# Expert 0 with two tiles at least: tiles 0 and 1 written out ahead of the expert loop

## The reference

```python
# 1. clustered attention: q, k, v are (2, 8, 768, 64); 16 cluster centroids per head
q_assign = argmax(normalised(q) . normalised(centroids));  k_assign likewise
mask = q_assign[:, :, :, None] == k_assign[:, :, None, :]
attn = softmax(where(mask, q @ k.T / 8, -1e9));  x = (attn @ v)   # -> (1536 tokens, 512)

# 2. mixture of experts: 8 experts, w1 (8, 512, 1024), w2 (8, 1024, 512)
logits = x @ w_gate;  e_idx = argmax(logits, axis=1)
gate_w = softmax(logits)[token, e_idx];  eom = sigmoid(x @ w_output_gate)
for e in range(8):
    mask = e_idx == e
    out[mask] = gate_w * eom[mask, e] * (relu(x[mask] @ w1[e]) @ w2[e])

# 3. dense part: w_in (512, 2048), w_out (2048, 512)
h = out @ w_in;  return (h * sigmoid(1.702 * h)) @ w_out
```

## Time and profile before

| | us |
|---|---|
| time, median of 3 runs (lowest to highest) | 813.9 (813.64 to 814.22) |
| time of the profiled execution | 814.3 |
| its span | 812.8 |
| TensorE matmuls busy | 748.0 (92%) |
| TensorE weight loads busy | 639.9 (79%) |
| VectorE busy | 425.5 (52%) |
| ScalarE busy | 371.4 (46%) |
| GpSimd busy | 164.8 (20%) |

### The profile page before, as it was taken

How to read it: one execution, slowest core, us unless ns; L and a number is a source line. 1 busy time by engine, 2 the same in 40 slices (tenths; PEclk the granted TensorE clock), 3 DMA queues, 4 the chain that set the end, 5 groups by cost and what they waited for, 6 DMA issues and landing times.

```text
span 812.8 us, 12003 instructions
## 1 busy us (share of the span) xinstructions
PE 748.0 (92%) x4099; PEld 639.9 (79%) x4099; DVE 425.5 (52%) x791; ACT 371.4 (46%) x707; POOL 164.8 (20%) x254
## 2 busy tenths in 40 slices
PE   4799999999999992879999999999999999999994
PEld 3699899988988871768777878888888888888883
DVE  3587888889878763455555546453322212222221
ACT  2577777777776840456565646463111101110110
POOL 5232242222635874101010101010000100020001
PEclk9999999999999996989999999999999999999997
DMA  7672552835526535773645364250000100010001
GB/s 173 153 167 69 135 123 65 184 71 129 150 55 136 212 130 129 235 261 117 234 141 205 124 234 181 67 191 18 1 0 1 53 0 1 1 52 0 1 1 52
DMA packets 61330, 86.36 MB, mean 106 GB/s; under 512 B 32576, under 2 KB 34768, under 8 KB 60752
## 3 DMA queue, kind: packets, MB, share of 16 engines
q1 hardware_dynamic: 55728, 75.23, 32.7%
q0 software_dynamic: 3376, 6.35, 2.2%
q10 hardware_dynamic: 2160, 3.93, 1.4%
HBM read 56.01 MB, written 9.05 MB: 80 GB/s over the span
## 4 chain that ended last, share of the span: by engine, by line
PE 71%; DVE 5%; ACT 5%; issue 5%; SPq 4%; DMA 3%; POOL 3%; ACTq 2%; another core or an unknown queue 0%; POOLq 0%; DVEq 0%
PE ps L958 16%; PE ps L686 9%; PE ps L973 5%; PE ps L975 5%; PE ps L974 5%; PE ps L759 5%; PE ps L901 4%; PE ps L903 3%; PE ps L902 3%; PE ps L888 3%; SPq L394 3%; PE ps L890 3%; PE ps L889 3%; PE ps L736 2%; PE ps L732 2%
## 5 line engine op out<-in xcount | busy, mean ns | idle before, releaser
L1341 DVE TENSOR_TENSOR pt_l<-ps,pt_h 128x384 fp32r<-128x384 f32 x192 | 105.9, 552 | 41.6 <-ACT pt_h L1062 40.1
L1210 ACT ACTIVATE g<-ps 128x512 f32<-128x512 f32 x48 | 28.7, 598 | 205.4 <-PE ps L958 205.4
L1571 DVE CAST gt_h<-g 128x512 fp32r<-128x512 f32 x48 | 20.5, 427 | 179.9 <-ACT g L1210 179.9
L1062 ACT CAST pt_h<-ps 128x384 fp32r<-128x384 f32 x192 | 92.6, 483 | 43.5 <-PE ps L686 43.5
L686 PE MATMUL ps<-ident,probs 128*128 128x128 f32 x576 | 97.3, 278 | 3.9 <-DVE pt_l L1341 2.2
L1300 DVE TENSOR_REDUCE nmax<-ps 128x1 f32<-128x768 f32 x96 | 91.0, 948 | 7.2 <-PE ps L736 7.2
L1033 ACT ACTIVATE probs<-ps,nmax 128x768 f32<-128x768 f32 x96 | 87.7, 913 | 4.8 <-DVE nmax L1300 4.8
L686 PEld LDWEIGHTS ps<-ident,probs 128*128 128x128 f32 x576 | 70.8, 144 | 17.7 <-ACT probs L1033 4.2
L958 PE MATMUL ps<-x2t_h,wl 128*128 128x512 f32 x192 | 74.9, 390 | 0.1
L973 PE MATMUL ps<-wh,gt_l 128*128 128x512 f32 x192 | 74.8, 389 | 0.0
L958 PE MATMUL ps<-x2t_h,wh 128*128 128x512 f32 x192 | 74.7, 389 | 0.0
(11 more groups left out here) (197 smaller groups left out, 1451.7 us busy)
## 6 DMA issues: line engine op xcount, KB each, us to landing
raw<-in_moe_w SPq DMA_DIRECT2D x32, 1024.0 KB, 7.7
ka<-hi_t SPq DMA_DIRECT2D x32, 192.0 KB
raw<-in_moe_w_in SPq DMA_DIRECT2D x4, 1024.0 KB, 5.9
raw<-in_moe_w_out SPq DMA_DIRECT2D x4, 1024.0 KB, 6.8
xg<-xs ACTq DMA_DIRECT2D x15, 256.0 KB, 3.9
qn<-in_q SPq DMA_DIRECT2D x16, 192.0 KB, 3.8
kn<-in_k SPq DMA_DIRECT2D x16, 192.0 KB, 3.9
vn<-in_v SPq DMA_DIRECT2D x8, 384.0 KB, 5.2
```

What stands on the lines that cost most here:

```text
L1062: nc.scalar.copy(pt_h[g % 2][:, half * GT:(half + 1) * GT, t3 * P:(t3 + 1) * P], ps[:, 4 + half, 0:GQ].rearrange("p (c n) -> p c n", c=GT) ...
L1341: nc.vector.tensor_tensor(pt_l[g % 2][at_p], ps[:, 4 + half, 0:GQ].rearrange("p (c n) -> p c n", c=GT), pt_h[g % 2][at_p].bitcast(F32), AL ...
```

## The change

Expert 0's minimum for the tiles after its first becomes one, so that it has two tiles always. With that, tile 0 and the first layer of tile 1 need no counts: they are written out straight on TensorE, ScalarE and VectorE with constant rows, and the loop starts at expert 1 (or at expert 0's third tile). The counts' chain is cut in parts (`count_tiles`, `region_rows`, `dense_rows`) that are put between VectorE's other work, each with a semaphore (`g_tiles`, `g_region`, `g_rows`). The pads have a semaphore for each expert; SP writes pad 0, fetches tile 1 by a constant row, writes pads 1 and 2, and the others one by one in the loop. POOL fetches tile 0's gate weights during attention (`first_info`). The second set of rank matmuls stands inside tile 0's first layer, and its totals have a bank column and a semaphore of their own (`g_total`).

```diff
@@ -340,16 +345,16 @@
         def expert_loop(eng, counter, tile, only=None):
 
             for e in range(E):
-                n = eng.value_load(ntiles[0:1, e:e + 1], min_val=1, max_val=MAXT)
-                tile(eng.snap(counter) if e else None, e, 0)
+                n = eng.value_load(ntiles[0:1, e:e + 1], min_val=1 if e else 2, max_val=MAXT)
                 if e:
+                    tile(eng.snap(counter), e, 0)
                     eng.reg_add(counter, counter, 1)
-                if only is not None:
-                    with eng.If(n < 2):
-                        only(e)
-                with eng.If(n > 1):
-                    tile(eng.snap(counter), e, 1)
-                    eng.reg_add(counter, counter, 1)
+                    if only is not None:
+                        with eng.If(n < 2):
+                            only(e)
+                    with eng.If(n > 1):
+                        tile(eng.snap(counter), e, 1)
+                        eng.reg_add(counter, counter, 1)
                 with eng.If(n > 2):
                     with eng.Fori(2, n):
                         tile(eng.snap(counter), e, 2)
...
             def fill(e):
 
                 n = sp.value_load(filled[0:1, e:e + 1], min_val=0, max_val=N)
-                return sp.dma_start(xs[bass.ds(n + e * REGION, TILE), :], zeros[:, :])
-
+                sp.dma_start(xs[bass.ds(n + e * REGION, TILE), :], zeros[:, :]).then_inc(s_pad[e], 16)
+
+            sp.wait_ge(g_filled, 1)
+            fill(0)
+            sp.wait_ge(s_pad[0], 16)
+            sp.wait_ge(s_disp, 16 * NT)
+            sp.dma_start(xg[:, :], xs[TILE:2 * TILE, :]).then_inc(xg_in, 16)
+            fill(1)
+            sp.wait_ge(pv_done, PAIRS * NG)
+            sp.wait_ge(g_rows, 1)
+            fetch_second(1)
+            fill(2)
             sp.wait_ge(g_tiles, 1)
-            row = sp.value_load(region_row[0:1, 2:3], min_val=0, max_val=E * REGION)
-            sp.wait_ge(s_disp, 16 * NT)
-            for e in range(2):
-                fill(e).then_inc(s_first, 16)
-            sp.wait_ge(s_first, 48)
-            fetch(row)
-            for e in range(2, E):
-                fill(e).then_inc(s_fill, 16)
-            sp.wait_ge(pv_done, PAIRS * NG)
-            fetch_second(1)
             tiles = sp.alloc_register("sp_tiles")
-            sp.reg_mov(tiles, 0)
+            sp.reg_mov(tiles, 1)
 
             def expert_tile(p, e, k):
 
-                g = 0 if p is None else p + 1
-                if k == 0 and e:
-                    sp.wait_ge(h_ready, 2 * g)
+                if k == 0:
+                    if e + 2 < E:
+                        fill(e + 2)
+                    sp.wait_ge(h_ready, 2 * (p + 1))
                     fetch_first(e + 1)
-                    sp.wait_ge(y_ready, g)
+                    sp.wait_ge(y_ready, p + 1)
                     fetch_second(e + 1)
 
...
+            def first_info():
+
+                pool.wait_ge(s_info, 16 * T)
+                nc.gpsimd.dma_start(scale[:, :], row_info[0:TILE, :]).then_inc(sc_in, 16)
+                nc.gpsimd.dma_start(sorted_info[0:TILE, :], row_info[0:TILE, :]).then_inc(s_sorted, 16)
...
-            n = pool.value_load(ntiles[0:1, E:E + 1], min_val=E, max_val=MAXT)
-            with pool.Fori(0, n) as p:
+            pool.wait_ge(s_sorted, 16)
+            n = pool.value_load(ntiles[0:1, E:E + 1], min_val=E + 1, max_val=MAXT)
+            with pool.Fori(1, n) as p:
...
@@ -785,11 +796,11 @@
                 for d in range(a + n - 1, 0, -1):
                     skip = max(0, d - a)
                     nc.tensor.matmul(dst[:, skip * E:], ones[:, :], picked[:, (a + skip - d) * E:(z - d) * E], start=False, stop=False)
-                last = nc.tensor.matmul(dst, before[:, :], picked[:, a * E:z * E], start=False, stop=True)
+                nc.tensor.matmul(dst, before[:, :], picked[:, a * E:z * E], start=False, stop=True).then_inc(g_rank, 1)
                 if st != 1:
                     for t in range(z):
-                        last = nc.tensor.matmul(ps[:, bank, col + n * E:col + n * E + E], ones[:, :], pick_b[:, t, :], start=(t == 0), stop=(t == z - 1))
-                last.then_inc(g_rank, 1)
+                        last = nc.tensor.matmul(ps[:, 7, TOTAL:TOTAL + E], ones[:, :], pick_b[:, t, :], start=(t == 0), stop=(t == z - 1))
+                    last.then_inc(g_total, 1)
...
-            hidden(0, 0, 0)
+            hidden(0, 0, 0, 0, 3)
             pe.wait_ge(g_row, 2)
             ranks(2)
+            hidden(0, 0, 0, 3)
+            hidden(0, 0, 1, 0, 1)
             hidden_transpose(0, 0)
-            hidden(0, 0, 1)
+            hidden(0, 0, 1, 1)
+            down(0, 0, 0)
+            hidden_transpose(0, 1)
+            down(0, 0, 2)
+            down(0, 0, 4)
+            down(0, 0, 6)
+            turned(0)
+            tile_transpose(1)
+            pe.wait_ge(xtl_done, 2)
+            hidden(1, 0, 0)
+            hidden(1, 0, 1, 0, 1)
+            hidden_transpose(1, 0)
+            hidden(1, 0, 1, 1)
 
             pe.wait_ge(g_tiles, 1)
             tiles = pe.alloc_register("pe_tiles")
-            pe.reg_mov(tiles, 0)
+            pe.reg_mov(tiles, 1)
 
             def expert_tile(p, e, k):
 
-                if p is None:
-                    return
                 g, ep = p + 1, e if k else e - 1
...
-            gate_exps(1)
-            relu(0, 0)
-            high(0, 0)
-            relu(0, 1)
...
-            def fetch(row):
-                act.wait_ge(s_fill, 32 + 16 * (E - 2))
+            def fetch(row, e):
+                act.wait_ge(s_pad[e], 16)
                 act.dma_start(xg[:, :], xs[bass.ds(row, TILE), :]).then_inc(xg_in, 16)
...
+            gate_exps(1)
+            relu(0, 0)
+            high(0, 0)
+            split_first(1, 0)
+            relu(0, 1)
+            high(0, 1)
+            for i in range(1, 4):
+                split_first(1, i)
+            scaled(0)
+            act.wait_ge(s_disp, 16 * NT)
+            turned_high(0, 0)
+            tile_high(1)
+            act.wait_ge(g_region, 1)
+            fetch(region_row_of(2), 1)
+            relu(1, 0)
+            high(1, 0)
+            relu(1, 1)
+            act.wait_ge(g_tiles, 1)
+            act.wait_ge(g_rows, 1)
+            tiles = act.alloc_register("act_tiles")
+            act.reg_mov(tiles, 1)
+
             def expert_tile(p, e, k):
 
-                if p is None:
-                    return
                 g = p + 1
                 split = split_second if k == 0 else split_first
                 whose = e if k == 0 else e + 1
                 row, ahead_row = row_at(p + 1), region_row_of(g + 1)
                 tile_high(g)
-                fetch(ahead_row)
+                fetch(ahead_row, min(e + 1, E - 1))
...
+            def total(st):
+
+                dve.wait_ge(g_total, 1 + st // 2)
+                nc.vector.tensor_copy(count[:, 1:SEG], ps[:, 7, TOTAL:TOTAL + E]).then_inc(g_count, 1)
+
             def place(st):
 
                 own = slice(*STAGES[st])
                 n = STAGES[st][1] - STAGES[st][0]
                 bank, at_c = (5, (st - 1) * GT * E) if st else (7, 3 * P)
                 dve.wait_ge(g_rank, st + 1)
-                if st != 1:
-                    nc.vector.tensor_copy(count[:, 1:SEG], ps[:, bank, at_c + n * E:at_c + n * E + E]).then_inc(g_count, 1)
+                if st == 0:
+                    total(st)
                 nc.vector.tensor_tensor(rank[:, own, :], ps[:, bank, at_c:at_c + n * E].rearrange("p (t e) -> p t e", e=E), pick_b[:, own, :], ALU.mult).then_inc(g_row, 1)
                 dve.wait_ge(g_row, st + 1)
                 link(nc.vector.reduce_sum(posf[:, own], rank[:, own, :], AX.X), g_step)
                 nc.vector.tensor_copy(pos[:, own], posf[:, own]).then_inc(g_ready, 1)
+                if st == 2:
+                    total(st)
...
+            def count_tiles():
...
+            def region_rows():
...
+            def dense_rows():
...
-
-
             dve.wait_ge(g_count, 2)
             nc.vector.tensor_copy(filled[:, 1:E], count[:, 2:SEG])
-            nc.vector.tensor_tensor(filled[:, 0:1], count[:, 1:2], gap[:, 1:2], ALU.add)
+            nc.vector.tensor_tensor(filled[:, 0:1], count[:, 1:2], gap[:, 1:2], ALU.add).then_inc(g_filled, 1)
             low(0, 0)
+            count_tiles()
+            low(0, 1)
+            region_rows()
+            split_first(1, 0)
             gate(1, 0)
             gate(1, 1)
+            turned_low(0, 0)
+            tile_low(1)
+            dense_rows()
+            split_first(1, 1)
+            split_first(1, 2)
+            low(1, 0)
+            split_first(1, 3)
+
+            dve.wait_ge(g_tiles, 1)
             dve.wait_ge(g_rows, 1)
             tiles = dve.alloc_register("dve_tiles")
-            dve.reg_mov(tiles, 0)
+            dve.reg_mov(tiles, 1)
```

(41 more changed lines are left out.)

62 lines of the change are left out of this document (24 added, 38 removed).

## The result

The changed kernel takes 808.9 us in the median of 12 runs (806.34 to 812.05), where the kernel before took 814.1 beside it (12 runs, 812.76 to 819.66): ratio 0.9933, 95% interval 0.9913 to 0.9953. That is faster, by a third of the 14.6 us forecast, and outside the range of 793 to 806. The profiled execution took 811.05 us, its span 809.6; it is one of the slower of the twelve, 2.1 us above their median.

A forecast was written before the change was run, and what follows sets the result against it. TensorE bounds the kernel, idle for 17.73 of the handover's 44.57 us; 24.1 work, 5.05 idle and 0.8 clock make 29.95, 14.6 less. Profiled 814.3 becomes 799.7, median 799.3; forecast 797 to 802, range 793 to 806.

The forecast's parts named there:

- The handover: From tile 0's first layer to tile 2's: 29.95 us against 44.57, as 24.1 work, 5.05 idle and 0.8 clock.
- the clock term: In the stretch up to tile 2's first layer, 0.8 us taken for lower clock, out of nothing to 2.7.
- Tile 1's fetch: Tile 1's input fetch goes out with a constant row at 311.65 and lands 4.3 us later, at 316.0.
- tile 2's first layer: On TensorE, starts at about 329.0 after 1.25 us of idle, behind ScalarE's register loads and copy.
- next in line: At tile 1's start: if its fetch lands earlier, VectorE's counts, region rows, split and gates hold it until 317.1.
- The late starts put down to instruction supply: VectorE's count copy (305.35) and ScalarE's copy (305.41) start late again at the same place; gain taken as 0.
- ScalarE's first ReLU: In tile 0's first layer, runs 304.1 to 304.7, covered by the second half's matmuls but for 0.1 us.
- ScalarE's wait for pad 2: Behind expert 1's 2 MB: issued about 321.3, lands 329 to 330.4, copy needed by 330.6; cost zero, barely.
- rival (b): New wait: fetch +3.2, pad 2 or scale +1 to +2, or stall 4 to 5; 802 to 806; chance 0.16.
- The scale: Tile 1's scale fetch goes out between 330 and 335.5, late by 0 to 5 us but covered; cost 0, bound 1.
- The jump: At expert 1's jump over two tile bodies, TensorE's 5 us gap is still there, at about 339.
- the pads' chain: Before tile 1's input: SP's waits for scattered rows and pads, then its fetch, stand behind 11.41 us of TensorE idle.

The follow-up runs named there:

- run 4: Changed kernel with POOL's six 8-byte scatters held until expert 1's second-layer weights have landed, SP's order untouched: 815.2 us, 1.0015 of the kernel before.
- run 5: Changed kernel with rows of row_info, token_info and scale widened from 8 to 64 bytes: 803.0 us, 0.9856 of the kernel before.
- run 1: Changed kernel with pad 2 written right behind pad 1, ahead of expert 1's second-layer weights: 807.97 us, 0.9924 of the kernel before.
- run 2: Changed kernel with pads 1 to 7 all written behind tile 1's input fetch, none in the loop: 803.9 us, 0.9885 of the kernel before.
- run 11: Changed kernel with all pads early, code for expert 1's third and further tile left out: 805.6 us, 0.9876 of the kernel before.
- run 12: Changed kernel with all pads early and 64-byte rows, TensorE's further tiles of an expert in one loop: 800.3 us, 0.9821 of the kernel before.
- run 3: Changed kernel with all pads early, batch 1's gates moved ahead of tile 0's low part so scatters come earlier: 810.5 us, 0.9958 of the kernel before.

## Why the prediction was wrong

The forecast for the profiled execution was 799.7; it took 811.05. Of the 11.4 us between them, 1.1 lie in the handover, 8.8 between tile 2's first layer and the matmul behind the jump, 1.5 later. By medians the forecast is missed by 9.6 us (799.3 against 808.9), since this execution was slower than most.

**The handover was right, by sum more than by term.** 31.09 us against 29.95. Busy time was 25.3 (24.9 with the clock term), idle time 5.8 (5.05). The clock stayed full throughout (0.8 had been allowed). Tile 1's fetch went out at 310.68 (311.65 forecast), tile 2's first layer at 330.90 (329.0). In the middle TensorE waited for VectorE, which the prediction had next in line, but its reason was another: not the counts and gates, which were done at 317.36, but tile 0's turned copies. `x2t_l` waited for ScalarE's `x2t_h`, and `xt_l` stood behind it. That the terms came out so near in sum is partly luck. VectorE's timeline:

```profile
302.71 0.18 DVE L1449 TENSOR_TENSOR rank<-ps,pick_b 128x24 f32<-128x24 f32 x1 [0.92 <-PE ps L799]
...
304.89 0.17 DVE L1439 COPY count<-ps 128x8 f32<-128x8 f32 x1 [1.58 <-remote]
...
307.70 0.69 DVE L1497 TENSOR_TENSOR ht_l<-ps,ht_h 128x512 fp32r<-128x512 f32 x1 [2.38 <-ACT ht_h L1145]
...
317.86 0.69 DVE L1553 TENSOR_TENSOR x2t_l<-ps,x2t_h 128x512 fp32r<-128x512 f32 x1 [0.51 <-ACT x2t_h L1160]
318.47 0.68 DVE L1491 TENSOR_TENSOR xt_l<-ps,xt_h 128x512 fp32r<-128x512 f32 x1
```

**The late starts put down to instruction supply: half right.** The stall stayed with the instruction that it had hit, the count copy (304.89; 305.35 in the earlier trace rows), but the rank product now stands ahead of it and ran 2.7 us earlier; the last row scatter went out at 307.90 and not 308.83. ScalarE's first ReLU came at 304.94, 0.8 later than my 304.1: TensorE idled 1.12 us there, where 0.1 was taken. That the supply of instructions is the cause was assumed; no run tests it.

**The pad: the step that failed.** "ScalarE's wait for pad 2: issued after expert 1's 2 MB at about 321.3, it lands 7.7 to 9.1 later", and then "Zero, barely." It was issued at 322.48 and landed at 338, after 15.5 us. In the profiled execution that cost 6.06 us of idle time and 2.9 us at the lower clock, where the sum had nothing. The landing times were taken from the pads of the kernel before as if they belonged to pads, and the cover ended at the upper end of the range. The prediction moved the scatters over the weights and the pad and priced only their own lateness. Runs 4 and 5 show what stood in its place: hold the scatters, or give them 64-byte rows, and the pad is in time with SP's order unchanged (2.4 and at most 8.4 us to landing). Run 1 shows that the pad was only the first to be late; without it the scale and the weights are. Its median is not told apart from the changed kernel's, so how much of the 6.06 us a typical execution pays is not known. So the size "+1 to +2" of rival (b) was the wrong one, not its kind.

**The scale.** Its fetch went out at 339.60, where 330 to 335.5 was forecast. It cost nothing in the changed kernel, where TensorE's matmuls, delayed by the pad, released tile 1's scaling last (345.56). In runs 1, 2 and 11 it cost TensorE 1.2, 1.5 and 3.8 us, more than the bound of 1.

The Trainium skill (DMA: Bandwidth & Descriptors, Queues, rings and completion order), which the prediction cited, has a completion wait for earlier writes of its DMA engine. That alone would let the scale wait for the weights whatever the row's size. With 64-byte rows POOL's idle time behind the last scatter was 7.70 us, with 8-byte rows 14.54. In both, 2.9 us of it are register loads. The wait itself is 4.8 and 11.6 us, so the rule can hold the 4.8 at most, and the larger part, 6.8 us, goes with the rows' width.

**The jump: right.** 4.98 us, 5.16 before. In runs 11 and 12 the jump passes over one body instead of two and the stall is gone, while it stayed between the kernel before and the changed one, whose code lies differently; that speaks for the distance jumped, though a shorter jump also moves the code. A page's rule bears on it: the Trainium skill (Runtime: NRT & Kernel Launch, Instruction fetch mechanics) says that a taken branch beyond what is loaded has to fetch its target. The packet records fit, with 16 KB for an instruction queue at 350.93 and TensorE going on at 354.24 (355.70 and 358.97 before). But that packet takes 1.0 us and starts only 4.1 us after the branch (346.80); what fills these 4.1 us is not shown.

**The later 1.5 us** stay open. They have arisen by the scaling of the last tile (539.01; 542.28 before), in steps of 0.4 us a tile at most; no run was made for them.

**Where the change's value went.** Against the kernel before: wide rows alone -0.57%, early pads alone -0.50%, both -1.04%; the change -0.67%, with 64-byte rows -1.44%, with all pads early too -1.58%, with TensorE's one loop -1.79%. Neither of the last two is told apart from the one ahead of it. With wide rows on both sides the change brings 0.9% (give or take 0.35), some 7 us of the 14.6. Another 0.57%, 4.6 us, is what wide rows alone bring: the handover's idle time, which the prediction put down to the pads' chain, was in part the scatters' doing. Together, the change with 64-byte rows is 11.7 us below the kernel before, 2.9 short of the forecast. In its profile the handover takes 32.85 us (297.98 to 330.83), 2.9 over the forecast 29.95, and the stretch behind it 14.38, as before the change. That its profiled execution took 801.33 us, only 1.6 over the forecast 799.7, is in part luck: attention ended 1.9 us earlier in it. What keeps the rest was not isolated; in run 12, without the stall, it is VectorE's splits that TensorE waits for.

## What to carry to other kernels

A transfer's time to landing, read from one profile, belongs to what was in flight beside it: when a change moves small scatters, price again every transfer that they now lie over. Look at GB/s next to the DMA engines' busy share; a high share with few GB/s is the sign. And a stall ahead of a late engine is cover, as in run 11: sum up what ends next before you book its removal.

## What the hardware showed

- Indirect scatters with 8 bytes a row slowed all DMA for 10 us and more: 135 GB/s where 64-byte rows left 295 at the same busy share of 0.82 (318 to 336), 64 packets of 2 KB over 1 us (up to 2.4) instead of 2. Rows of 32 bytes were as good as 64 (803.1 and 803.0 us). The Trainium skill (Collectives: The Full Stack, Rules for kernel authors) asks, for the buffers of collectives, for an alignment to 32 bytes, to prevent a read-modify-write. These scatters are no collectives; rows of 32 bytes also start at multiples of 32 bytes in their buffer, so the runs fit a limit at or below 32 bytes, but don't tell size from alignment or show what happens underneath.
- In run 3, with the scatters early, ScalarE stood for 2.77 and 5.14 us beside the slow phase; the cause is not shown.
- A TensorE branch over two tile bodies took 5.0 to 6.6 us in every profile that has it; in runs 11 and 12, where none passes over more than one body, the longest took 0.37.
